# Three edits to a fused attention, soft MoE and ELU FFN kernel: how w1 is cut into loads, the order of the head's loads, and the order of the slots' softmax

## The chip, the cores and the metric

The kernel runs on one core of one Trainium2 chip. The metric is device time in microseconds (us), median of three runs. A profiled execution of the same kernel supplies the trace that is read below.

## The reference: what is computed

Three stages follow one another. Every array is float32.

```python
# 1: recurrent linear attention, B=4, H=8, S=768, D=48
for t in range(S):
    cur = np.einsum('bhd,bhe->bhde', u[None] * kt, vt)
    y[:, :, t] = np.einsum('bhd,bhde->bhe', rt, state + cur)
    state = w[None, :, :, None] * state + np.einsum('bhd,bhe->bhde', kt, vt)
# 2: soft MoE over x = y as [3072, 384]; 8 experts of 4 slots, w1[e] is 384x1024, w2[e] 1024x384
logits = x @ phi                       # [3072, 32]
d = softmax(logits, axis=0); slot_input = d.T @ x
h = np.maximum(slot_input[e] @ w1[e], 0.0); slot_out[e] = h @ w2[e]
x = softmax(logits, axis=1) @ slot_out
# 3: x @ w_in (384x2048), ELU, @ w_out (2048x384)
```

## The kernel before

**Attention.** The sequence is cut into 6 chunks of 128 tokens and each chunk into 4 units, one per batch entry, so there are 24 units. For each unit GpSimd (POOL) scales k into `k_nat` and makes the products r·u·k, TensorE (PE) turns k and r (`turn_k`, `turn_r`), makes scores, state terms and values, VectorE (DVE) evacuates with the decay tables, ScalarE (ACT) writes diagonals and y. Engines are synchronised by semaphores written by hand, and each engine runs its instructions in the order of the code.

**Loads.** Nearly all loads are issued by SyncE (SP) on one queue, called q1 in the profile, in program order. r, k and v come in rows of 48 numbers (192 bytes): each `load` call issues three transfers, one of 192 KB over 128 partitions and two of 96 KB over 64. `load_chunk` issues, for each half chunk, v, then k and r of the next chunk, then one piece of w1 (`load_w1`). w1 of one expert is 128 rows of 12 KB, one row to each partition: before the change it is cut across the row, into an 8 KB piece (two thirds, 1 MB) and a 4 KB piece (one third, 512 KB), both over all 128 partitions. The eight large pieces are loaded during attention, two small ones in the head, and the six others in the last chunk. Behind these, on the same queue, come w2 (`load_w2`, eight loads of 1.5 MB), w_in (two loads) and w_out (four). The profile shows w1 as `w_sb`, w2 as `w`.

**Head.** Before the first unit, w is loaded into `wcol`, raised to powers by repeated squaring in `wpow`, and `tables_T` holds w^t and w^-t. `wpow[:, 6]` is w^64 and `wpow[:, 7]` is w^128.

**Slots' softmax.** The softmax over the 3072 tokens runs in a turned layout. Chunks 0 to 4 are exponentiated early, with the maximum so far; the last chunk gets a new maximum (`neg_top[:, 1]`), its own exponentials `exp_T`, and a rescale of the earlier sum. PE turns the maxima (line 799) and `exp_T` (line 806), sums weighted tokens with `slot_in(c)`, and after `den_cols`, `fold_w` and `slot_parts` comes `slot_T`, which the experts' first matmul (`expert_in`, line 826) reads. It also waits for all of w1.

**FFN.** `expert_out` waits for w2 expert by expert; `G_first` and `G_others` multiply the 32 slots by w_in (line 903 needs w_in's second piece), ACT rounds w_out (line 1387), `move_G` moves parts of G_T from one group of 32 partitions to another, and a long stretch of matmuls (lines 976 to 978) ends the kernel.

Of the kernel before, what the change touches and what calls it, by code (L numbers as in the profile page):

```python
# [36 lines left out]
def attention_moe_ffn_kernel(nc, r, k, v, w, u, phi, w1, w2, w_in, w_out, out):  # L37
# [22 lines left out]
    with ExitStack() as ctx:  # L60
# [68 lines left out]
        logits_T = place("logits_T", [P, CHUNKS, P], F32)  # L129
# [86 lines left out]
        ps_warm = banks[5][:, 0:P]  # L216

# [174 lines left out]
        def _(sp):  # L392
# [44 lines left out]
            load_w1(range(2), slice(2, KD))  # L437
# [151 lines left out]
        def _(pe):  # L589
# [399 lines left out]
        def _(dve):  # L989
# [10 lines left out]
            for n in range(6):  # L1000
# [3 lines left out]
                dve.tensor_tensor(wpow[:, n + 1, :, :], wpow[:, n, :, :], wpow[:, n, :, :], ALU.mult).then_inc(powers, 1)  # L1004
# [46 lines left out]
            def logits_T_to_sbuf(c):  # L1051
# [5 lines left out]
                dve.tensor_copy(logits_T[:, c, :], logits_now[:, :]).then_inc(lT_kept, 1)  # L1057
# [88 lines left out]
            def row_weights(units):  # L1146
# [14 lines left out]
            logits_to_sbuf(CHUNKS - 1)  # L1161
# [5 lines left out]
            dve.wait_ge(exp_turned, 2)  # L1167
            dve.tensor_copy(col_w[:, EARLY_CHUNKS * B:UNITS, :].rearrange("p b s -> p (b s)"), banks[1][:, P:2 * P]
                            ).then_inc(col_w_ready, 1)
            dve.wait_ge(act_step, A_FOLD)  # L1170
            dve.tensor_tensor(fold_w[:, 1, :], fold_w[:, 1, :], fold[:, :], ALU.mult).then_inc(dve_step, 1)
            row_inverses(EARLY)
# [4 lines left out]
                              banks[3][:, DM:DM + 1].broadcast_to([P, P]), ALU.add).then_inc(dve_step, 1)  # L1177
            dve.tensor_tensor(slot_parts[:, :, :], *(x[:, 0:DM].rearrange("p (q c) -> p c q", c=KD) for x in (slot_early, banks[3])),
# [13 lines left out]

# [273 lines left out]
```

## Time and profile before

| | |
|---|---|
| median of 3 runs | 394.32 us (394.05 to 395.26) |
| profiled execution, its own time | 392.18 us |
| its span in the trace | 390.4 us |
| PE busy | 374.2 us (96%) |
| DVE, ACT, POOL busy | 69%, 56%, 26% |
| HBM read | 45.86 MB |
| granted TensorE clock | 1.00 |

The profiled execution took 1.78 us beyond its span, and the median of the three runs is 2.14 us above the profiled execution. A wait is read from the timeline rows: what stands in brackets is how long the engine idled before the group of instructions, and what released it. The DMA view gives, for a stretch, packets, megabytes, and the time that packets took as a share of 16 engines times the stretch.

### The profile page before, as it was taken

Reading aid. Unit: us, or ns where it says so; the run is one execution under the profiler, and the core shown is the slowest. Engines: PE = TensorE matmul, PEld = TensorE weight load, DVE = VectorE, ACT = ScalarE, POOL = GpSimd, SP = SyncE. Lnnn points to the kernel's source line nnn. Section 1 sums busy time; section 2 is a strip of 40 time slices with the busy share of each in tenths; the row PEclk is TensorE's granted clock in tenths of the full one; section 3 lists DMA queues with packets and bytes.
Section 4 is the critical chain, followed back from the end, with each engine's and each line's share of the span. In section 5 each row is a group of like instructions: output and inputs, shape, how many; then the busy total and the mean of one; then the engine's idle time right before and its main releaser. Section 6 shows DMA issues by size and latency. Waiting matters only on the chain.

```text
span 390.4 us, 11439 instructions
## 1 busy us (share of the span) xinstructions
PE 374.2 (96%) x4373; PEld 333.0 (85%) x4373; DVE 267.6 (69%) x512; ACT 219.6 (56%) x498; POOL 103.3 (26%) x136
## 2 busy tenths in 40 slices
PE   6898999999889999999999999999999999999996
PEld 3787898989775454589999999999999999999996
DVE  4787788778767620699867767667777667776671
ACT  2896778777772131588564446444644464455441
POOL 7797777777640000355200000000000000000000
PEclk9999999999999999999999999999999999999999
DMA  7989899999999999920020002000200020002002
GB/s 152 254 151 186 199 234 233 227 255 254 235 303 426 430 432 403 373 64 2 0 83 1 2 0 81 0 0 0 81 0 0 0 81 0 0 0 82 2 2 81
DMA packets 87280, 51.80 MB, mean 133 GB/s; under 512 B 77776, under 2 KB 83024, under 8 KB 85200
## 3 DMA queue, kind: packets, MB, share of 16 engines
q1 hardware_dynamic: 82368, 50.21, 43.1%
q10 hardware_dynamic: 4880, 1.16, 1.4%
q8 instruction: 19, 0.31, 0.3%
q14 instruction: 13, 0.11, 0.1%
HBM read 45.86 MB, written 4.72 MB: 130 GB/s over the span
## 4 chain that ended last, share of the span: by engine, by line
PE 79%; DMA 10%; SPq 3%; issue 3%; ACT 3%; DVE 1%; POOL 1%; DVEq 0%; POOLq 0%; ACTq 0%
PE psum L976 17%; PE psum L978 17%; PE psum L977 17%; PE psum L911 6%; DMA w_out_raw<-in_moe_w_out_dram 4%; PE psum L603 4%; DMA r_raw<-in_r_dram 3%; PE psum L643 3%; PE psum L826 3%; PE psum L686 3%; PE psum L667 2%; PE psum L656 2%; PE psum L696 2%; DMA v_sb<-in_v_dram 1%; PE psum L703 1%
## 5 line engine op out<-in xcount | busy, mean ns | idle before, releaser
L978 PE MATMUL psum<-w_out_hi,elu_lo 128*128 128x384 f32 x372 | 125.8, 338 | 0.0
L976 PE MATMUL psum<-w_out_hi,elu_hi 128*128 128x384 f32 x372 | 125.7, 338 | 0.0
L977 PE MATMUL psum<-w_out_lo,elu_hi 128*128 128x384 f32 x372 | 125.3, 337 | 0.0
L1405 ACT ACTIVATE exp_h<-psum 128x512 f32<-128x512 f32 x96 | 57.6, 600 | 97.3 <-PE psum L911 97.0
L1246 DVE SCALAR_TENSOR_TENSOR elu<-psum,neg_part 128x512 f32<-128x512 f32 x96 | 66.3, 690 | 57.1 <-ACT neg_part L1392 57.1
L977 PEld LDWEIGHTS psum<-w_out_lo,elu_hi 128*128 128x128 f32 x372 | 69.8, 188 | 3.9
L976 PEld LDWEIGHTS psum<-w_out_hi,elu_hi 128*128 128x128 f32 x372 | 70.4, 189 | 0.0
L978 PEld LDWEIGHTS psum<-w_out_hi,elu_lo 128*128 128x128 f32 x372 | 69.9, 188 | 0.0
L1238 DVE TENSOR_TENSOR elu_lo<-elu,elu_hi 128x512 fp32r<-128x512 f32 x96 | 66.3, 691 | 0.6
L1280 ACT ACTIVATE scores<-ident_wide,bonus 128x128 f32<-128x128 f32 x192 | 58.8, 390 | 5.0 <-DVE bonus L1028 4.9
L1392 ACT ACTIVATE neg_part<-exp_h 128x512 f32<-128x512 f32 x96 | 60.0, 626 | 1.7 <-DVE elu L1246 1.3
L1259 DVE CAST elu_hi<-elu 128x512 fp32r<-128x512 f32 x96 | 44.0, 458 | 0.6
L1041 DVE COPY_PREDICATED scores<-mask,psum 128x512 f32<-128x512 uint32 x48 | 33.3, 736 | 15.3 <-PE psum L643 12.9
L911 PE MATMUL psum<-c_T,G_T 128*128 (+1 forms) x96 | 37.6, 397 | 0.8 <-DMA G_T<-G_parts 0.6
L686 PE MATMUL psum<-scores,v_sb 64*64 64x128 f32 (+1 forms) x768 | 25.9, 245 | 1.8 <-issue 1.6
L527 POOL TENSOR_TENSOR k_nat<-k_raw,k_table 128x384 f32<-128x384 f32 x23 | 23.2, 1009 | 15.6 <-PE psum L667 7.9
L584 POOL TENSOR_TENSOR w_out_lo<-w_out_raw,w_out_hi 128x384 fp32r<-128x384 f32 x16 | 16.8, 1058 | 34.4 <-ACT w_out_hi L1387 34.4
L686 PEld LDWEIGHTS psum<-scores,v_sb 64*64 64x64 f32 x768 | 22.4, 133 | 2.8 <-issue 2.8
L538 POOL TENSOR_TENSOR k_raw<-k_raw,r_raw 128x384 f32<-128x384 f32 x22 | 22.1, 1006 | 6.0 <-DMA r_raw<-in_r_dram 4.7
L643 PE MATMUL psum<-r_pair,k_pair 48*64 48x128 f32 (+1 forms) x768 | 20.9, 245 | 1.8 <-DVE r_pair L1035 1.8
L535 POOL TENSOR_TENSOR k_raw<-k_raw,u_row 128x384 f32<-128x384 f32 x22 | 22.1, 1006 | 1.7
L911 PEld LDWEIGHTS psum<-c_T,G_T 128*128 128x128 f32 x96 | 18.1, 190 | 3.5 <-issue 1.7
(155 smaller groups left out, 403.6 us busy)
## 6 DMA issues: line engine op xcount, KB each, us to landing
w<-in_moe_w_dram SPq DMA_DIRECT2D x8, 1536.0 KB, 13.6
w_sb<-in_moe_w_dram SPq DMA_DIRECT2D x8, 1024.0 KB, 6.3
out_dram<-out_sb SPq DMA_DIRECT2D x24, 192.0 KB, 1.9
w_sb<-in_moe_w_dram SPq DMA_DIRECT2D x8, 512.0 KB, 6.2
w_out_raw<-in_moe_w_out_dram SPq DMA_DIRECT2D x4, 768.0 KB, 15.7
r_raw<-in_r_dram SPq DMA_DIRECT2D x12, 192.0 KB, 3.2
r_raw<-in_r_dram SPq DMA_DIRECT2D x24, 96.0 KB, 3.4
w_in_sb<-in_moe_w_in_dram SPq DMA_DIRECT2D x1, 2304.0 KB, 19.4
```

Source lines behind the costliest of these rows:

```text
L686: m = pe.matmul(ps_y[e * HP:e * HP + HP, two, q * P + cols.start:q * P + P], v_sb[rows, q, b, 2 * e + two, :], scores[rows, i, h, cols], s ...
L911: pe.matmul(banks[4 + f % RING][:, :], G_T[:, f * P:(f + 1) * P], c_T[:, bass.ds(i * BANK, BANK)], start=True, stop=True).then_inc(ffn_don ...
L976: pe.matmul(acc, hi, w_out_hi[:, f, :], start=(f == 0), stop=False)
L977: pe.matmul(acc, hi, w_out_lo[:, f, :], start=False, stop=False)
L978: m = pe.matmul(acc, lo, w_out_hi[:, f, :], start=False, stop=(f == KF2 - 1))
L1041: dve.copy_predicated(scores[:, i, two::2, :].rearrange("p (n a) t -> p n a t", n=2), mask[:, :, :].bitcast(U32).unsqueeze(2).broadcast_to ...
L1238: dve.tensor_tensor(elu_lo[:, f % RING, :], elu[:, f % 2, :], elu_hi[:, f % RING, :].bitcast(F32), ALU.subtract).then_inc(lo_done, 1)
L1246: dve.scalar_tensor_tensor(out=elu[:, f % 2, :], in0=banks[4 + f % RING][:, :], scalar=0.0, in1=neg_part[:, f % 2, :], op0=ALU.max, op1=AL ...
L1259: dve.tensor_copy(elu_hi[:, f % RING, :], elu[:, f % 2, :]).then_inc(hi_done, 1)
L1280: m = act.activation(scores[:, i, h, :], ident if h < H // 2 else ident_swap, ACT.Copy, scale=bonus[:, i, h:h + 1])
L1392: act.activation(neg_part[:, f % 2, :], exp_h[:, f % 2, :], ACT.Relu, bias=1.0, scale=-1.0).then_inc(neg_ready, 1)
L1405: act.activation(exp_h[:, f % 2, :], banks[4 + f % RING][:, :], ACT.Exp).then_inc(exp_done, 1)
```

## The change

There are three edits.

- **w1's pieces.** `load_w1` takes rows (partitions) instead of thirds. The first piece of an expert is partitions 0 to 79 with the whole 12 KB row (960 KB), the second partitions 80 to 127 (576 KB). Where they are issued, and in what number, stays.
- **The head.** SP issues u_row and then r; ACT issues the two loads of w, its table load and k, then v ahead of phi. Before, SP issued w and then r, and ACT k, u, phi and v. w^64 is written to PSUM (`w64`) instead of `wpow[:, 6]`; a copy of it and one more wait come ahead of w^128.
- **The slots' softmax.** PE turns `exp_T` right behind the maxima and moves the last chunk's turned logits (`chunk_logits`) behind `slot_in(5)`; DVE evacuates the exponentials first and moves the last logits and `row_inverses(EARLY)` behind `slot_T`; `exp_T` reads `logits_now` and the copy into `logits_T` is not made for the last chunk; on ACT `slot_early` goes ahead of the exponential of `fold_w`.

```diff
-            def load_w1(experts, thirds):
+            def load_w1(experts, rows):
                 for e in experts:
-                    sp.dma_start(w1_sb[:, e * KD + thirds.start:e * KD + thirds.stop, :], w1_dram[e][:, thirds, :]
-                                 ).then_inc(w1_loaded, 16)
+                    sp.dma_start(w1_sb[rows, e * KD:(e + 1) * KD, :], w1_dram[e][rows, :, :]).then_inc(w1_loaded, 16)
...
-                        load_w1([2 * (c - 1) + g], slice(0, 2))
+                        load_w1([2 * (c - 1) + g], slice(0, 5 * P // 8))
                     if last and g == 0:
-                        load_w1(range(2, E), slice(2, KD))
-            sp.wait_ge(cleared, 1)
-            for half in range(2):
-                sp.dma_start(wcol[half * HP:half * HP + D, :], w_cols, allow_slow_non_contiguous=True
-                             ).then_inc(w_loaded, 16)
+                        load_w1(range(2, E), slice(5 * P // 8, P))
+            sp.dma_start(u_row[:, :, :].rearrange("p h d -> p (h d)"), u_flat.broadcast_to([P, DM])).then_inc(u_loaded, 16)
             load_r(0, 0)
...
-            load_w1(range(2), slice(2, KD))
+            load_w1(range(2), slice(5 * P // 8, P))
...
             pe.transpose(banks[0][0:1, 0:P], neg_top[:, 1:2], ident[:, :]).then_inc(pe_step, 1)
-            chunk_logits(CHUNKS - 1)
+            pe.wait_ge(exp_T_ready, 2)
+            pe.transpose(banks[1][:, P:2 * P], exp_T[:, :], ident[:, :]).then_inc(exp_turned, 1)
             slot_in(2)
+            slot_in(3).then_inc(x_used, 1)
...
             slot_in(5).then_inc(pe_step, 1)
+            chunk_logits(CHUNKS - 1)
             keep_clock_up(2)
-            pe.wait_ge(dve_step, D_DENCOLS)
+            pe.wait_ge(dve_step, D_FOLD)
...
-                dve.tensor_tensor(wpow[:, n + 1, :, :], wpow[:, n, :, :], wpow[:, n, :, :], ALU.mult).then_inc(powers, 1)
+                dve.tensor_tensor(wpow[:, n + 1, :, :] if n < 5 else w64, wpow[:, n, :, :], wpow[:, n, :, :], ALU.mult).then_inc(powers, 1)
...
-            dve.tensor_tensor(wpow[:, 7, 0, :], wpow[:, 6, 0, :], wpow[:, 6, 0, :], ALU.mult).then_inc(powers, 1)
+            dve.tensor_copy(wpow[:, 6, 0, :], w64[:, 0, :]).then_inc(powers, 1)
+            dve.wait_ge(powers, 16)
+            dve.tensor_tensor(wpow[:, 7, 0, :], wpow[:, 6, 0, :], w64[:, 0, :], ALU.mult).then_inc(powers, 1)
...
+            act.wait_ge(cleared, 1)
+            for half in range(2):
+                act.dma_start(wcol[half * HP:half * HP + D, :], w_cols, allow_slow_non_contiguous=True
+                              ).then_inc(w_loaded, 16)
+            act.wait_ge(cleared, 2)
+            act.activation(exp_warm[:, :], v_sb[:, 0, 0, 0, D:D + 1], ACT.Exp)
             load(act, k_raw, k_dram, 0, 0, k_loaded)
-            act.wait_ge(const_set, 5)
-            act.activation(exp_warm[:, :], ident[:, 0:1], ACT.Exp)
-            act.dma_start(u_row[:, :, :].rearrange("p h d -> p (h d)"), u_flat.broadcast_to([P, DM])).then_inc(u_loaded, 16)
...
+            load(act, v_sb, v_dram, 0, 0, v_loaded)
+            act.wait_ge(powers, 15)
+            act.copy(tables_T[:, 1, 2:PAIRS, 0:HP], tables_T[:, 1, 2:PAIRS, HP:P]).then_inc(table_swapped, 1)
```

SP's instructions in the order of the program, first the head, before the change (`w_sb` is w1, the last numbers are partitions x elements):

```order
L430 DMA wcol<-in_w_dram 48x8x1 x2
L375 DMA r_raw<-in_r_dram 128x8x48
L376 DMA r_raw<-in_r_dram 64x8x48
L377 DMA r_raw<-in_r_dram 64x8x48
L375 DMA k_raw<-in_k_dram 128x8x48
```

The same place on SP in the changed kernel:

```order
L429 DMA u_row<-in_u_dram 128x384
L377 DMA r_raw<-in_r_dram 128x8x48
L378 DMA r_raw<-in_r_dram 64x8x48
L379 DMA r_raw<-in_r_dram 64x8x48
L377 DMA k_raw<-in_k_dram 128x8x48
```

w has left SP's queue for ACT's, and u stands in its place; r is issued second as before.

SP in the last chunk and behind it, before:

```order
L377 DMA v_sb<-in_v_dram 64x8x48
L405 DMA w_sb<-in_moe_w_dram 128x1024 x6
L441 DMA w_0_84<-in_moe_w_dram 128x3072
L441 DMA w_1_85<-in_moe_w_dram 128x3072
L441 DMA w_2_86<-in_moe_w_dram 128x3072
```

And in the changed kernel:

```order
L379 DMA v_sb<-in_v_dram 64x8x48
L407 DMA w_sb<-in_moe_w_dram 48x3072 x6
L439 DMA w_0_84<-in_moe_w_dram 128x3072
L439 DMA w_1_85<-in_moe_w_dram 128x3072
L439 DMA w_2_86<-in_moe_w_dram 128x3072
```

The six pieces stand in the same place, ahead of w2. Their shape went from 128 partitions of 1024 numbers to 48 partitions of 3072.

PE in the slots' softmax, from the turned maxima to the experts, before:

```order
L799 MATMUL psum<-ident_wide,neg_top 1x128
L709 MATMUL psum<-ident_wide,logits_now 128x128
L725 MATMUL psum<-x_sb,col_w 32x386 x4
L803 MATMUL psum<-top_row,ones 128x32
L806 MATMUL psum<-ident_wide,exp_T 128x128
L725 MATMUL psum<-x_sb,col_w 32x386 x12
L593 MATMUL psum<-ones 128x128 x2
L812 MATMUL psum<-fold_w,den_cols 128x32
```

And in the changed kernel:

```order
L797 MATMUL psum<-ident_wide,neg_top 1x128
L799 MATMUL psum<-ident_wide,exp_T 128x128
L723 MATMUL psum<-x_sb,col_w 32x386 x8
L803 MATMUL psum<-top_row,ones 128x32
L723 MATMUL psum<-x_sb,col_w 32x386 x8
L707 MATMUL psum<-ident_wide,logits_now 128x128
L591 MATMUL psum<-ones 128x128 x2
L810 MATMUL psum<-fold_w,den_cols 128x32
```

The exponentials' turn moved ahead of all of `slot_in(2)` to `slot_in(5)`, and the logits' turn behind them; the number of matmuls is the same.

## Rows read from the trace of the kernel before

**Rows 1.** The page: granted clock and GB/s in 40 slices of 9.76 us

```profile
PEclk9999999999999999999999999999999999999999
...
GB/s 152 254 151 186 199 234 233 227 255 254 235 303 426 430 432 403 373 64 2 0 83 1 2 0 81 0 0 0 81 0 0 0 81 0 0 0 82 2 2 81
```

**Rows 2.** The chain that ended last: start us, us, what

```profile
77.74 5.56 DMA v_sb<-in_v_dram
...
93.25 4.04 DMA r_raw<-in_r_dram
...
102.86 4.50 DMA r_raw<-in_r_dram
...
144.50 16.14 DMA w_out_raw<-in_moe_w_out_dram
```

**Rows 3.** Timeline of SP's queue: start us, us, line, output<-input

```profile
66.77 0.62 SPq L405 DMA_DIRECT2D w_sb<-in_moe_w_dram  x1
...
103.54 0.66 SPq L405 DMA_DIRECT2D w_sb<-in_moe_w_dram  x1
...
107.77 5.94 SPq L405 DMA_DIRECT2D w_sb<-in_moe_w_dram  x6
```

**Rows 4.** Timeline of POOL in attention, with the idle time before it

```profile
76.40 1.01 POOL L527 TENSOR_TENSOR k_nat<-k_raw,k_table 128x384 f32<-128x384 f32 x1 [1.89 <-DMA k_raw<-in_k_dram]
```

**Rows 5.** The DMA view of 119 to 150 us: totals, share of 16 engines

```profile
DMA packets 1386, 13.21 MB, mean 426 GB/s; under 512 B 144, under 2 KB 144, under 8 KB 359
...
q1 hardware_dynamic: 1382, 13.15, 100.4%
```

**Rows 6.** The DMA view of 111.4 to 118.6 us, the last w1 pieces

```profile
DMA packets 740, 2.68 MB, mean 372 GB/s; under 512 B 91, under 2 KB 91, under 8 KB 738
```

**Rows 7.** The DMA view of 169.95 to 170.45 us, one G_T move, 40 slices

```profile
GB/s 0 0 0 164 492 328 164 0 164 164 328 0 328 328 164 0 328 492 655 164 164 0 0 164 164 0 164 0 164 1 2 164 0 0 0 1 0 0 0 0
...
q1 hardware_dynamic: 48, 0.07, 55.5%
```

**Rows 8.** The DMA view of 388 to 390.4 us, the last stores

```profile
q1 hardware_dynamic: 398, 0.54, 63.3%
```

**Rows 9.** Timeline where the FFN begins: start us, us, engine, line, operation

```profile
158.84 1.92 PE L903 MATMUL psum<-w_in_sb,slot_out_T 128*32 128x512 f32 x12 [0.66 <-DMA w_in_sb<-in_moe_w_in_dram]
...
160.67 0.93 ACT L1387 CAST w_out_hi<-w_out_raw 128x384 fp32r<-128x384 f32 x2 [2.62 <-DMA w_out_raw<-in_moe_w_out_dram]
```

**Rows 10.** Timeline of the head

```profile
0.95 1.03 SPq L430 DMA_DIRECT2D wcol<-in_w_dram  x2
...
2.02 0.47 SPq L375 DMA_DIRECT2D r_raw<-in_r_dram  x1
...
6.12 0.39 SPq L375 DMA_DIRECT2D k_raw<-in_k_dram  x1
...
7.53 0.15 DVE L1022 TENSOR_TENSOR wpow<-wpow 128x4 f32<-128x4 f32 x1
...
7.95 0.63 PE L603 MATMUL psum<-ident_wide,r_raw 128*128 128x128 f32 x4 [1.73 <-DMA r_raw<-in_r_dram]
...
17.75 0.51 POOL L566 TENSOR_TENSOR state<-state_sum,wpow 128x192 f32<-128x192 f32 x1
```

**Rows 11.** Timeline of the slots' softmax and after it

```profile
122.06 0.86 PE L725 MATMUL psum<-x_sb,col_w 128*32 128x386 f32 x8
...
123.18 0.33 PE L806 MATMUL psum<-ident_wide,exp_T 128*128 128x128 f32 x1
...
125.70 0.29 DVE L1176 TENSOR_TENSOR den_cols<-slot_early,psum 128x128 f32<-128x128 f32 x1 [0.42 <-PE psum L725]
...
127.97 3.59 PE L826 MATMUL psum<-w_sb,slot_T 128*32 128x512 f32 x29
...
131.99 1.75 DVE L1202 TENSOR_TENSOR row_parts<-row_w,row_hi 128x1536 fp32r<-128x1536 f32 x1
...
139.24 1.45 PEld L861 LDWEIGHTS psum<-ident_r,row_parts 128*128 128x128 f32 x16
```

More of the change, by code:

```diff
@@ L127, in attention_moe_ffn_kernel @@
         W1_END = cursor[0]
-        logits_T = place("logits_T", [P, CHUNKS, P], F32)
+        logits_T = place("logits_T", [P, CHUNKS - 1, P], F32)
         exp_T = place("exp_T", [P, P], F32)
@@ L216, in attention_moe_ffn_kernel @@
         ps_warm = banks[5][:, 0:P]
+        w64 = banks[1][:, 0:2 * PAIRS].rearrange("p (n a) -> p n a", n=2)
         h_banks = ((banks[3], banks[4]), (banks[0], banks[7]))
@@ L341, in attention_moe_ffn_kernel @@
         LOADED = 3 * 16
-        DECAY_SET = 16
+        DECAY_SET = 17
         PE_TOP_T, PE_TOP_ROWS, PE_SLOT_IN, PE_DEN, PE_SLOT_T = range(1, 6)
-        (D_TOP_ROW, D_FOLD_SHIFT, D_FOLD, D_DENCOLS, D_SLOT_PARTS, D_DENEPS, D_DENINV, D_SLOT_T,
+        (D_TOP_ROW, D_FOLD_SHIFT, D_DENCOLS, D_FOLD, D_SLOT_PARTS, D_DENEPS, D_DENINV, D_SLOT_T,
          D_ROWW, D_ROWW_LATE, D_ROWHI, D_PARTHI, D_PARTLO) = range(1, 14)
-        A_RESCALE, A_FOLD, A_EARLY_SLOTS, A_IDENT_R = range(1, 5)
+        A_RESCALE, A_EARLY_SLOTS, A_FOLD, A_IDENT_R = range(1, 5)
         def move_G(eng, n, j):
@@ L804, in _ @@
                       ).then_inc(pe_step, 1)
-            pe.wait_ge(exp_T_ready, 2)
-            pe.transpose(banks[1][:, P:2 * P], exp_T[:, :], ident[:, :]).then_inc(exp_turned, 1)
-            slot_in(3).then_inc(x_used, 1)
             slot_in(4).then_inc(early_slots_done, 1)
             slot_in(5).then_inc(pe_step, 1)
+            chunk_logits(CHUNKS - 1)
             keep_clock_up(2)
-            pe.wait_ge(dve_step, D_DENCOLS)
+            pe.wait_ge(dve_step, D_FOLD)
             pe.matmul(banks[0][:, 2 * P:2 * P + SLOTS], den_cols[:, :], fold_w[:, 1, :], start=True, stop=True
@@ L1014, in _ @@
                 dve.tensor_tensor(tables_T[:, n, pairs, 0:HP], tables_T[:, n, pairs, HP:P],
-                                  wpow[:, 6, 1 - n, pairs].unsqueeze(2).broadcast_to([P, pairs.stop, HP]), ALU.mult
+                                  w64[:, 1 - n, pairs].unsqueeze(2).broadcast_to([P, pairs.stop, HP]), ALU.mult
                                   ).then_inc(tables_done, 1)
@@ L1056, in logits_T_to_sbuf @@
                 dve.tensor_reduce(chunk_top[:, c:c + 1], logits_now[:, :], AX.X, ALU.max).then_inc(chunk_top_ready, 1)
-                dve.tensor_copy(logits_T[:, c, :], logits_now[:, :]).then_inc(lT_kept, 1)
+                if c < EARLY_CHUNKS:
+                    dve.tensor_copy(logits_T[:, c, :], logits_now[:, :]).then_inc(lT_kept, 1)
             def early_top():
@@ L1160, in _ @@
                               ).then_inc(dve_step, 1)
-            logits_to_sbuf(CHUNKS - 1)
+            dve.wait_ge(exp_turned, 2)
+            dve.tensor_copy(col_w[:, EARLY_CHUNKS * B:UNITS, :].rearrange("p b s -> p (b s)"), banks[1][:, P:2 * P]
+                            ).then_inc(col_w_ready, 1)
             dve.wait_ge(pe_step, PE_TOP_ROWS)
@@ L1166, in _ @@
                               ).then_inc(dve_step, 1)
[L1167 to L1172, printed above, removed]
             dve.wait_ge(pe_step, PE_SLOT_IN)
@@ L1177, in _ @@
                               banks[3][:, DM:DM + 1].broadcast_to([P, P]), ALU.add).then_inc(dve_step, 1)
+            dve.wait_ge(act_step, A_FOLD)
+            dve.tensor_tensor(fold_w[:, 1, :], fold_w[:, 1, :], fold[:, :], ALU.mult).then_inc(dve_step, 1)
             dve.tensor_tensor(slot_parts[:, :, :], *(x[:, 0:DM].rearrange("p (q c) -> p c q", c=KD) for x in (slot_early, banks[3])),
@@ L1191, in _ @@
                                   ).broadcast_to([P, KD, E, SPE]), ALU.mult).then_inc(dve_step, 1)
+            logits_to_sbuf(CHUNKS - 1)
+            row_inverses(EARLY)
             row_weights(EARLY)
@@ L1302, in _ @@
                                   ).then_inc(phi_loaded, 16)
-            act.wait_ge(powers, 15)
-            act.copy(tables_T[:, 1, 2:PAIRS, 0:HP], tables_T[:, 1, 2:PAIRS, HP:P]).then_inc(table_swapped, 1)
-            load(act, v_sb, v_dram, 0, 0, v_loaded)
             act.wait_ge(table_turned, 1)
@@ L1345, in _ @@
             act.wait_ge(top_ready, 2)
-            act.wait_ge(lT_kept, CHUNKS)
-            act.activation(exp_T[:, :], logits_T[:, CHUNKS - 1, :], ACT.Exp, bias=neg_top[:, 1:2]).then_inc(exp_T_ready, 1)
+            act.wait_ge(lT_ready, CHUNKS)
+            act.activation(exp_T[:, :], logits_now[:, :], ACT.Exp, bias=neg_top[:, 1:2]).then_inc(exp_T_ready, 1)
             act.activation(rescale[:, :], neg_top[:, 0:1], ACT.Exp, bias=neg_top[:, 1:2], scale=-1.0).then_inc(act_step, 1)
-            act.wait_ge(dve_step, D_FOLD_SHIFT)
-            act.activation(fold_w[:, 1, :], fold_w[:, 0, :], ACT.Exp).then_inc(act_step, 1)
             act.wait_ge(early_slots_done, 1)
@@ L1353, in _ @@
             act.activation(slot_early[:, :], banks[2][:, 0:DM + 2], ACT.Copy, scale=rescale[:, :]).then_inc(act_step, 1)
+            act.wait_ge(dve_step, D_FOLD_SHIFT)
+            act.activation(fold_w[:, 1, :], fold_w[:, 0, :], ACT.Exp).then_inc(act_step, 1)
             act.wait_ge(rows_shifted, 2)
```

2 lines of the change are left out of this document (1 added, 1 removed).

## The prediction, made before the changed kernel was timed

> **What bounds the kernel now.** I began with the page's slices [rows 1]: the granted clock is full (2.4 GHz) all through, and from the 12th slice to the 17th the DMA moves 303 to 432 GB/s. The chain that ended last [rows 2] tells where that matters. It runs through a load of w_out from 144.50 us, 16.14 us long, which ends when the FFN can begin, and during attention through v and r. So I split the kernel in three.
>
> Until about 107 us it is attention. Its second half runs to the beat of SP's queue: w1's pieces are issued at 66.77 and, four pieces later, at 103.54 [rows 3], so 9.2 us for half a chunk, and POOL waits for k at each (1.89 us in the row shown, and four waits like it from 67 to 104 us) [rows 4]. In this stretch, time that a w1 piece takes on the queue delays the k, r and v behind it.
>
> From 107.77 us, when the last six pieces of w1 are issued [rows 3], the queue is full. From 111.4 to 118.6 us it moves 372 GB/s in 4 KB rows [rows 6], then 426 GB/s in the 12 KB rows of w2 [rows 5]. w_in's second piece and w_out's first end the stage: PE waits 0.66 us for the one and ACT 2.62 us for the other, until 160.67 us [rows 9]. Every microsecond that the queue loses between 111 and 160 us is a microsecond of the kernel. The softmax and the experts lie beside it; after 160.67 us PE is busy to the end, and nothing of the change is there.
>
> **w1's pieces, last stage.** The six second pieces go from 6 x 0.524 = 3.15 MB over 128 partitions to 6 x 0.590 = 3.54 MB over 48. Before, at 372 GB/s [rows 6], they cost 8.5 us. What does a transfer cost that lands in a part of the partitions? The nearest rows are the moves of G_T, 64 KB from 32 partitions to 32. One fills slices 4 to 32 of 40, 29 x 0.0125 = 0.36 us, so 181 GB/s while it runs [rows 7], though all 16 engines share it. Its packets took 55.5% x 16 x 0.5 us = 4.44 us of engine time for 65.5 KB, or 14.8 GB/s per engine. The last stores, in packets of 1.5 KB over 128 partitions, took 63.3% x 16 x 2.4 = 24.3 us for 0.54 MB, or 22.2 GB/s per engine [rows 8]; w2 took 100.4% x 16 x 31 = 498 us for 13.15 MB, or 26.4 GB/s per engine [rows 5]. The shorter packets of the stores are faster than those of G_T, so the length does not explain it: few partitions do. The bounds for 3.54 MB are then 8.3 us (426 GB/s, no loss), 15.0 us (G_T's engine rate, 16 x 14.8 = 236), 19.6 us (181) and 22.1 us (160, which is 426 in proportion to 48 of 128 partitions). The last two are the nearest in kind, since the first ignores the row and the second leaves out that the engines wait unevenly. I take 21 us: **+12.5**.
>
> The Trainium skill speaks against this edit: SBUF — State Buffer, section Door 1: The DMA port swizzle, says that the partitions hang on 16 ports of 27.2 GB/s, eight to each, and that a range of partitions gets only the ports it reaches. By its map, four ports hold eight of the partitions 80 to 127 each, so a piece would need 8 x 12 KB / 27.2 GB/s = 3.6 us and six 21.7 us, which is an estimate from that page; the sum would be 0.7 us higher. The G_T moves agree with it, at 181 GB/s against its 218 for 32 partitions; no run before shows an HBM load of this shape.
>
> Who waits: w1 would be complete near 111 + 21 + 2 = 134 us instead of 111 + 8.5 = 119.5, so `expert_in`, which began at 127.97 [rows 11], begins some 6 us late. w2 is queued behind and later by 12.5, so PE waits for each expert, and w_in and w_out arrive 12.5 later.
>
> **w1's pieces in attention.** The eight first pieces go from 1.049 MB (2.5 us at 426) to 0.983 MB over 80 partitions: 2.3 us without loss, 3.7 us at 80/128 of the rate (266 GB/s), so between -0.2 and +1.2 us each. At 181 GB/s, G_T's own, it would be 5.4 us, +2.9; I take +1.2, since 80 partitions are far more than 32. From 66.77 to 103.54 us there are these four beats that the queue sets [rows 3, 4], so +4.9 there; the earlier pieces have slack or half of it. In the head the two second pieces cost 2 x 2.2 us more of queue time at 14 to 20 us, where PE has its data well ahead; I put 0 there, up to +2. With a little taken back by later slack: **+5** (from -1 to +9).
>
> **The head.** r's issue moves from 2.02 us to about 1.3, since SP no longer waits for w's two issues of 1.03 us, but k's on ACT moves back by about the same, behind them. PE's first turn needs r (landed at 7.9 us) and its second k, which released SP at 6.12 [rows 10]. The bytes ahead of both are the same, so both land near 7.4: **-0.3**, between -0.8 and +0.8. w^64 in PSUM, its copy and one wait touch a chain that ends at 7.53 + 0.15 us, while POOL needs w^128 at 17.75 [rows 10]: 0. Without that cover it would be the copy, about 0.15 us, like the product in that row.
>
> **The softmax.** PE turned `exp_T` at 123.18, between `slot_in(2)`, which began at 122.06, and the other three [rows 11]; now it does so about 1 us sooner, but the four `slot_in` that follow take 0.86 us for the first and as much or less for each of the others, and there was hardly a gap between them. `den_cols` at 125.70 comes at best 0.5 us sooner. `row_parts`, 1.5 us later because `row_inverses` moved behind `slot_T`, would be ready at 131.99 + 1.75 + 1.5 = 135.2 against PE's use at 139.24 [rows 11]. All this lies beside the queue: **0**. If that cover were gone it would be worth -0.5.
>
> **Sum.** 392.18 (the profiled execution) + 12.5 + 5 - 0.3 = 409.4; the median lies 2.1 above the profiled one, so 411.5 us.
>
> **The rivals.**
> - *No loss by partitions* (0.16). G_T's packets also come out of 32 partitions of SBUF and are 2 KB; a load from HBM in 12 KB rows might not care. Then the last stage gains 8.5 - 8.3 = 0.2, attention loses 0.066 MB a beat, -0.15 to -0.3 each over four beats, and the head gives -0.3: 394.3 - 1.5 = 392.8. Faster decides from where 3.54 MB move at more than 3.54 / 9.8 = 361 GB/s, as the other gains are 1.3. For it speaks that 4 KB rows moved at 372 and 12 KB rows at 426 [rows 5, 6]; against it rows 7 beside rows 8. Of this, faster has 0.11 and same 0.05.
> - *Half of it* (0.12). The queue's engines run on without waiting for one another, so those with light rows take w2 early, and the price is G_T's engine rate: last stage 15.0 - 8.5 = +6.5, attention +2, head -0.3: 402.5. Against it: w_in and w_out need the slowest engine.
> - *The clock falls as well* (0.10). PE, busy all through now at full clock [rows 1], would wait for w2 expert by expert. If it were granted 1.2 GHz at the start of the FFN, line 903's 1.92 us and what follows until the first G_T moves would double, +3 to +5: 415.5. No row here is at that level.
>
> The forecast itself has 0.62, its own range 404 to 417.
>
> **How the numbers follow.** About 0.3% is what a measurement of this kernel can tell from no change. The range 398 to 419 holds the forecast, the half case and most of the clock case, 0.62 + 0.12 + 0.08, and leaves out the case without loss. Faster 0.11, same 0.05, slower 0.84.
>
> **What would show it.** In the profile after, w1's last pieces land 3.5 us apart and the GB/s fall to 150 to 200 from 111 to 132 us; PE waits for w1 before line 824 and then for w2; the beat of SP's pieces goes from 9.2 to 10.4 us; w_out lands near 178 us. If instead the GB/s stay at 400 behind the last v, the first rival is right and the prediction is wrong. If the softmax matters, PE's wait for w_in would have to be gone.

## The result and the profile after

The changed kernel takes 426.15 us (median of four runs, 424.39 to 428.64) against 394.79 us of the kernel before beside it: the ratio is 1.086, with an interval of 1.079 to 1.092. It is 31 us slower, 15 us more than forecast and outside the range.

The page of the changed kernel, granted clock and GB/s in 40 slices, here of 10.65 us, beside [rows 1]:

```profile
PEclk9988989989998799999999999999999999999999
...
GB/s 133 182 143 152 197 176 182 204 204 206 205 186 176 148 255 430 424 410 357 42 0 0 77 0 2 71 2 0 0 74 0 0 61 13 0 0 75 1 2 74
```

The queue is at 206 GB/s or less up to the 14th slice, where before it moved 227 to 303 from the 6th to the 12th. The clock, full before in every slice, drops under 90% in six of the first 14. From the 16th slice the rates are those of before.

The chain that ended last, beside [rows 2]:

```profile
24.74 5.58 issue
...
50.70 4.07 issue
...
71.17 6.39 DMA v_sb<-in_v_dram
...
91.99 6.62 DMA v_sb<-in_v_dram
...
133.08 24.25 DMA w_sb<-in_moe_w_dram
157.37 10.51 PE psum L824 x96
...
173.89 22.05 DMA w_out_raw<-in_moe_w_out_dram
```

New are two long stretches "issue", in which PE waited for nothing that the chain names (before, the longest was 1.38 us), and 24.25 us for w1. The wait for w_out went from 16.14 to 22.05 us.

SP's queue, beside [rows 3], with the first, the fourth and the eighth of the large pieces:

```profile
19.67 6.67 SPq L377 DMA_DIRECT2D r_raw<-in_r_dram  x1
...
44.07 1.13 SPq L407 DMA_DIRECT2D w_sb<-in_moe_w_dram  x1
...
79.65 0.34 SPq L407 DMA_DIRECT2D w_sb<-in_moe_w_dram  x1
...
122.90 0.62 SPq L407 DMA_DIRECT2D w_sb<-in_moe_w_dram  x1
...
125.81 7.69 SPq L407 DMA_DIRECT2D w_sb<-in_moe_w_dram  x6
```

[rows 3] has the fourth, at 66.77, and the eighth, at 103.54; the first stood here before:

```profile
35.92 0.62 SPq L405 DMA_DIRECT2D w_sb<-in_moe_w_dram  x1
```

The last six pieces are issued at 125.81 us instead of 107.77: **18.0 us** are lost by then. 8.2 of them are lost by the first large piece. From the first to the fourth it is three half chunks of 11.86 us (before 10.28), 4.7 us more; from the fourth to the eighth four of 10.81 us (before 9.19), 6.5 us more. Behind the eighth 1.3 us come back.

The end of the stage, beside [rows 9]:

```profile
157.37 10.51 PE L824 MATMUL psum<-w_sb,slot_T 128*32 128x512 f32 x96 [0.55 <-DMA w_sb<-in_moe_w_dram]
...
195.96 0.93 ACT L1392 CAST w_out_hi<-w_out_raw 128x384 fp32r<-128x384 f32 x2 [2.74 <-DMA w_out_raw<-in_moe_w_out_dram]
```

From the six pieces to this row it is 70.15 us instead of 52.90: **17.25 us** more. From it to the end it is 229.9 us, before 229.7. So the loss is 18.0 + 17.25 = 35.3 us, the difference of the spans (425.9 - 390.4 = 35.5; this profiled run took 427.61 us, the one of before 392.18, so they lie 4 us further apart than the medians).

The DMA view of 134 to 156 us, when the last w1 pieces move, and the same stretch by windows (PE, PEld, DVE, ACT, POOL busy, granted clock, DMA share, GB/s):

```profile
DMA packets 365, 3.46 MB, mean 157 GB/s; under 512 B 84, under 2 KB 84, under 8 KB 84
...
q1 hardware_dynamic: 363, 3.43, 99.0%
...
134.00:156.00 22.00, 15.60 (x199) 9.39 (x192) 7.07 (x17) 3.95 (x9) 0.82 (x1) 0.77 1.00 157
```

The DMA engines are busy 99% of the time, as with w2 before [rows 5], but move 157 GB/s instead of 426: their packets take longer. PE is busy for 15.60 of these 22 us. It idles only 0.55 us for w1; its long gap is another one, a stop of 6.11 us in the middle of a group:

```profile
146.73 1.08 PE L701 MATMUL psum<-y_T,phi_sb 128*32 128x128 f32 x15 [6.11 <-issue]
```

The granted clock averages 0.77 in the window (0.50 in the 2.3 us behind this stop), and 1.00 between 156 and 190 us. PE's 96 products for the experts take 10.51 us in both timelines, so here this fall of the clock cost them nothing.

The middle of the head and the first chunk, timeline rows with the idle time before them:

```profile
23.97 0.78 PE L641 MATMUL psum<-r_pair,k_pair 48*64 48x128 f32 x22
...
30.32 0.58 PE L641 MATMUL psum<-r_pair,k_pair 48*64 48x64 f32 x10 [5.58 <-issue]
...
30.13 1.00 POOL L525 TENSOR_TENSOR k_nat<-k_raw,k_table 128x384 f32<-128x384 f32 x1 [7.12 <-DMA k_raw<-in_k_dram]
```

PE stops after 22 of 32 matmuls of one group, without a wait that the trace names, and goes on 5.58 us later. The kernel before has one such stop above 1 us, 1.38 us at 32.65 us. POOL meanwhile waits for k.

### The profile page after: what moved, and what is told of

It is laid out like the page before. It is cut to its first block, busy times and chain, and to the rows that moved or that the text cites. A ratio compares the mean times of both kernels' runs of the same rounds, so it can differ in the third digit from the quotient of the medians.

```text
span 425.9 us, 11439 instructions
## 1 busy us (share of the span) xinstructions
PE 384.7 (90%) x4373; PEld 339.3 (80%) x4373; DVE 266.2 (62%) x512; ACT 219.7 (52%) x498; POOL 103.4 (24%) x136
## 3 DMA queue, kind: packets, MB, share of 16 engines
HBM read 45.86 MB, written 4.72 MB: 119 GB/s over the span
## 4 chain that ended last, share of the span: by engine, by line
PE 67%; DMA 17%; SPq 7%; issue 4%; POOL 2%; DVE 1%; ACT 1%; ACTq 0%; POOLq 0%; DVEq 0%
PE psum L974 15%; PE psum L976 15%; PE psum L975 15%; DMA w_sb<-in_moe_w_dram 6%; DMA w_out_raw<-in_moe_w_out_dram 5%; PE psum L909 5%; DMA v_sb<-in_v_dram 3%; PE psum L601 3%; SPq L377 3%; PE psum L824 2%; PE psum L641 2%; SPq L407 2%; PE psum L684 2%; SPq L378 2%; PE psum L665 2%
## 5 line engine op out<-in xcount | busy, mean ns | idle before, releaser
L1041 DVE COPY_PREDICATED scores<-mask,psum 128x512 f32<-128x512 uint32 x48 | 32.9, 734 | 27.2 <-PE psum L641 26.5
L684 PE MATMUL psum<-scores,v_sb 64*64 64x128 f32 (+1 forms) x768 | 27.3, 255 | 2.4 <-DMA v_sb<-in_v_dram 1.7
L641 PE MATMUL psum<-r_pair,k_pair 48*64 48x128 f32 (+1 forms) x768 | 21.9, 248 | 6.6 <-issue 5.6
L684 PEld LDWEIGHTS psum<-scores,v_sb 64*64 64x64 f32 x768 | 24.0, 141 | 3.7 <-issue 3.7
L641 PEld LDWEIGHTS psum<-r_pair,k_pair 48*64 48x64 f32 x768 | 19.4, 136 | 7.4 <-issue 7.2
L1276 ACT COPY k_pair<-psum 128x512 f32<-128x512 f32 x23 | 13.4, 584 | 19.9 <-PE psum L601 19.8
## 6 DMA issues: line engine op xcount, KB each, us to landing
w<-in_moe_w_dram SPq DMA_DIRECT2D x8, 1536.0 KB, 22.1
```

Of the source, the lines that this page charges most:

```text
L641: m = pe.matmul(ps_A[two][e0:e0 + HP, a, cols], k_pair[rows, i, a, e0:e0 + HP], r_pair[rows, i, a, cols], start=True, stop=True, skip_grou ...
L684: m = pe.matmul(ps_y[e * HP:e * HP + HP, two, q * P + cols.start:q * P + P], v_sb[rows, q, b, 2 * e + two, :], scores[rows, i, h, cols], s ...
```

## The experiments

Each was run beside the kernel before. All that differ in w1 alone are named "w1 edit alone" and keep the head and the softmax of before. The diffs of experiments 3, 4 and 7 are against the w1 edit alone, that of 5 against the cut at 64, that of 8 against the new head alone, the others against the kernel before. A profile is one execution, and single profiles scatter by some 2 us at a given row (experiment 2, softmax), so smaller differences in such rows aren't read as effects.

**1. Loads alone.** All computation is left out, and the output is zeros. Eight series of w1 loads and two of v, each awaited before the next; of the third:

```diff
...
+            for e in range(E):
+                sp.dma_start(w1_sb[80:128, e * KD:(e + 1) * KD, :], w1_dram[e][80:128, :, :]).then_inc(landed[2], 16)
+            sp.wait_ge(landed[2], 16 * E)
...
```

> This kernel leaves out all of the computation: it only issues series of eight loads of w1 into SBUF, waits for each series, then v's rows, then stores zeros. Each series is eight loads on SP's queue. Theory P (the partitions set the rate: a transfer gets a share of the way into SBUF by the partitions it lands in): 128 partitions run at about 425 GB/s with 12 KB rows and 370 to 410 with 4 KB rows; partitions 80 to 127 at 160 to 180 GB/s (8 x 0.59 MB in 26 to 29 us); partitions 0 to 79 at 210 to 270; 0 to 63 at 210 to 220; 0 to 31 at 180 to 220, so hardly less than 0 to 63; every other partition, also 64 of them but spread over all, clearly over 0 to 63, 300 to 425; 4 KB rows into partitions 80 to 127 also near 165. Rival R (the 12 KB row is what costs): whole experts over 128 partitions are as slow as the partial ones, and 4 KB rows into 48 partitions are fast. Rival N (the number of partitions counts, wherever they lie): every other partition is as slow as 0 to 63, and 0 to 31 takes half the rate of 0 to 63. For v's rows of 192 bytes P expects no difference between 128 partitions and two halves of 64.

SP's queue: each series of eight loads ends where the next begins.

```profile
2.14 3.97 SPq L250 DMA_DIRECT2D w_sb<-in_moe_w_dram  x8
14.90 3.98 SPq L254 DMA_DIRECT2D w_sb<-in_moe_w_dram  x8
47.13 3.65 SPq L258 DMA_DIRECT2D w_sb<-in_moe_w_dram  x8
81.34 3.81 SPq L262 DMA_DIRECT2D w_sb<-in_moe_w_dram  x8
118.08 5.09 SPq L266 DMA_DIRECT2D w_sb<-in_moe_w_dram  x8
151.00 4.99 SPq L270 DMA_DIRECT2D w_sb<-in_moe_w_dram  x8
168.65 3.57 SPq L274 DMA_DIRECT2D w_sb<-in_moe_w_dram  x8
185.73 3.57 SPq L278 DMA_DIRECT2D w_sb<-in_moe_w_dram  x8
197.63 13.43 SPq L282 DMA_DIRECT2D v_sb<-in_v_dram  x6
213.28 18.78 SPq L288 DMA_DIRECT2D v_sb<-in_v_dram  x12
234.40 12.17 SPq L294 DMA_DIRECT2D out_dram<-out_sb  x24
```

| series, partitions and row | MB | us | us a load | GB/s |
|---|---|---|---|---|
| L250: 0 to 127, 4 KB | 4.19 | 12.76 | 1.60 | 329 |
| L254: 0 to 127, 12 KB | 12.58 | 32.23 | 4.03 | 390 |
| L258: 80 to 127, 12 KB | 4.72 | 34.21 | 4.28 | 138 |
| L262: 0 to 79, 12 KB | 7.86 | 36.74 | 4.59 | 214 |
| L266: 0 to 63, 12 KB | 6.29 | 32.92 | 4.12 | 191 |
| L270: every other, 12 KB | 6.29 | 17.65 | 2.21 | 356 |
| L274: 0 to 31, 12 KB | 3.15 | 17.08 | 2.14 | 184 |
| L278: 80 to 127, 4 KB | 1.57 | 11.90 | 1.49 | 132 |

The times hold the start and the landing of a series, 1.4 to 2.3 us in which no w1 packet moves. The DMA views without them give 407 GB/s for 0 to 127, 147 for 80 to 127, 223 for 0 to 79, 206 for 0 to 63, 394 for every other and 207 for 0 to 31.

Sixty-four neighbouring partitions and sixty-four alternate ones have the same size of row, bytes and count, and differ by a factor of 1.9. So it is the place of the partitions, with the rows of w1 in HBM that belong to them: no run moves the one without the other, but the whole experts, read from neighbouring rows as well, aren't slow. A load of 48, 64 or 80 neighbouring partitions takes as long as one of all 128: **either piece of an expert costs as much as the whole expert**, 4.59 + 4.28 against 4.03 us. The 4 KB row is as slow by the byte as the 12 KB one (132 and 138 GB/s). So rivals R and N are out, and theory P has the order right, but several of its figures were too high (80 to 127: 138 instead of 160 to 180), and with v it failed: six loads of its 192-byte rows over 128 partitions, each awaited, take 15.65 us, and the same bytes as two halves of 64 take 21.12 us. Whether the place or the second load of each pair costs this isn't separated.

The Trainium skill, SBUF — State Buffer, section Door 1: The DMA port swizzle, has this pattern: each of the four sets 0 to 63, 0 to 79, 80 to 127 and 0 to 127 has some port with eight of its partitions, for which an estimate from that page's port rate is 8 x 12 KB / 27.2 GB/s = 3.6 us, and every other partition or 0 to 31 puts four on a port, 1.8 us by the same estimate. The runs agree in the order, and lie 12 to 27% above (4.03 to 4.59, and 2.14 to 2.21); without the start and the landing of the series it is 5 to 21% (3.83 to 4.38, and 1.90 to 1.99). It is the fullest port that fits, not the section's own rule of 27.2 GB/s for each port that a range reaches: that would be an estimate of 218 GB/s for 80 to 127 (eight ports) and 326 for 0 to 79 (twelve), against 147 and 223 in the DMA views.

**2. One edit at a time.** The kernel before with one of the three edits, each as in the diff of the change; of the first one:

```diff
-                        load_w1([2 * (c - 1) + g], slice(0, 2))
+                        load_w1([2 * (c - 1) + g], slice(0, 5 * P // 8))
```

> The kernel before with the edit to w1's pieces alone. If w1's pieces carry the whole loss, 424 us, within 2 of the changed kernel's 426.15, the granted clock again near 0.97, and PE idle for some 5 us in the third slice of 9.8 us. If the head and the softmax carry a part of it (rival H), 415 to 421 us.

> The kernel before with the new head alone (loads' order and w^64 in PSUM). In the changed kernel PE's first turn of r began at 9.27 us instead of 7.95, with w landed 1.6 us later. Theory: the new order itself does that, +1.3 us at the first turn, of which attention gives back some: 394.8 to 396.2 us. Rival: the late start is an accident of that one execution and the prediction's -0.3 holds: 394.0 to 394.5.

> The kernel before with the new order of the slots' softmax alone. The queue of w2, w_in and w_out ends the stage, so the forecast is no change, 394.3 plus or minus 0.5, with w_out landing at 160.7 as before although the experts begin up to 0.5 us sooner. Rival: the softmax lets w2's later loads be issued sooner and gives 0.5 us or more.

w1 alone: 424.26 us, ratio 1.084 (1.077 to 1.092). Head alone: 394.91 us, 1.010 (1.003 to 1.018). Softmax alone: 393.62 us, 1.002 (0.998 to 1.006), no change (its profiled run, 395.92, is the slowest of ten and has w_out at 164.38 us, not 160.7). The w1 edit carries the loss.

**3. Bytes moved, width kept.** The w1 edit alone, with the same 983 and 590 KB in each piece, but cut by columns over all 128 partitions.

```diff
-                    sp.dma_start(w1_sb[rows, e * KD:(e + 1) * KD, :], w1_dram[e][rows, :, :]).then_inc(w1_loaded, 16)
+                    sp.dma_start(w1_sb[:, :, :].rearrange("p (e c) f -> p e (c f)", e=E)[:, e, cols], w1_dram[e].rearrange("p c f -> p (c f)")[:, cols]).then_inc(w1_loaded, 16)
```

> The w1 edit alone with the same bytes in each piece (983 KB first, 590 KB last), but cut by columns over all 128 partitions: rows of 7.5 and 4.5 KB. Theory A, the loss is the partitions': no loss, the last six cost 0.39 MB more than before at about 400 GB/s, +1 us, attention -0.5: 394 +- 2 us. Theory B, that moving bytes from the first to the last pieces, or pieces that aren't whole rows of a third, costs it: over 400 us.

392.86 us, ratio 1.002 (0.998 to 1.005). Last pieces issued at 106.27 us (-1.5), from there to w_out 54.06 us (+1.2). Theory A: the split of the bytes costs nothing that this can tell.

**4. Half of the partitions, neighbouring or alternate.** The w1 edit alone, two kernels, of each the line of the first pieces (the last pieces take the other 64 partitions):

```diff
-                        load_w1([2 * (c - 1) + g], slice(0, 5 * P // 8))
+                        load_w1([2 * (c - 1) + g], slice(0, P // 2))
```

```diff
-                        load_w1([2 * (c - 1) + g], slice(0, 5 * P // 8))
+                        load_w1([2 * (c - 1) + g], slice(0, P, 2))
```

> The w1 edit alone, cut at partition 64 instead of 80: first pieces in partitions 0 to 63, last ones in 64 to 127, 786 KB each, the same count and the same 12 KB rows. In the loads alone 0 to 63 took 4.1 us each (191 GB/s) against 4.5 for 0 to 79 and 4.2 for 80 to 127. Theory A, the adjacent partitions share ways into SBUF: as slow as the cut at 80, beats of 10 to 11 us, the last six pieces about 24 us, 418 to 428 us in all. Theory B, it is the uneven cut, 5 to 3, that leaves some ways idle: the even cut gives back at least half of the loss, under 410 us.

> The w1 edit alone, but the first piece of an expert is its even partitions and the last its odd ones: 64 partitions, 786 KB, the same 12 KB rows and the same number of pieces as with the cut at 64. Theory A, place alone matters: 356 GB/s in the loads alone, so 2.2 us for a piece; the first pieces have 262 KB less than before (-0.6 us a beat over four beats, -2), the last six 1.57 MB more than before (4.72 MB at 356 = 13.3 us against 8.5, +4.8): 393 to 398 us, the granted clock back at 1.00 and the stalls of PE with the releaser issue under 1.5 us. Theory B, that few partitions or rows of 12 KB in a part of the tile are slow wherever they lie: over 415 us, as with the cut at 64.

Neighbouring: 418.42 us, ratio 1.069 (1.062 to 1.076). Alternate: 393.98 us, 1.005 (1.002 to 1.008). Clock and GB/s of the alternate cut:

```profile
PEclk9998999999999999999999999999999999999999
...
GB/s 151 254 162 172 195 222 217 233 243 204 229 363 425 426 431 407 383 82 2 0 82 2 2 0 80 0 0 0 80 0 0 0 80 0 0 0 82 2 2 80
```

Against 155 to 208 GB/s of the neighbouring cut in slices 3 to 14, this is nearly the kernel before. With rows, bytes and counts of the same size the place is worth 24 us. PE has one stop above 1 us, 1.60 us, slightly over the 1.5 expected. The 1.57 MB more in the last stage fit what remains of 0.5%: the issue comes at 105.78 us (-2.0), w_out 2.95 us later than before from there.

In the cut at 64 the clock had a price: the 96 products of the experts begin at 147.29 us, run at a granted clock of 0.50 until 152 us, and take 13.46 us instead of 10.51.

**5. Does a neighbour in the queue fill the idle ways?** The cut at 64, with the next piece in the opposite half.

```diff
-                        load_w1([2 * (c - 1) + g], slice(0, P // 2))
+                        load_w1([2 * (c - 1) + g], slice(g * HP, g * HP + HP))
...
-                        load_w1(range(2, E), slice(P // 2, P))
+                        for e in range(2, E):
+                            load_w1([e], slice((1 - e % 2) * HP, (1 - e % 2) * HP + HP))
```

> The cut at partition 64 as in the run of that cut (418.4 us), but neighbours in the queue lie in opposite halves: of an even expert the first piece is 0 to 63 and the last 64 to 127, of an odd one the other way round. Theory A, the engines stay on the same piece, so it is narrow whatever its neighbour: 416 to 421 us. Theory B, the engines run a piece or more apart, so that opposite halves fill all the ways: the last six go from 24 us towards the 13.3 of every other partition, the head's two pieces too, and the kernel takes 398 to 410 us.

418.79 us, ratio 1.065 (1.059 to 1.071), the same as without. From the last six pieces to w_out it is 68.36 us, against 68.79. Theory A: a neighbour in the other half gives nothing back.

**6. The two stages apart.** The kernel before, with wide pieces issued as two halves of 64 partitions, in attention only, or in the last stage only.

```diff
+                    for half in halves:
+                        sp.dma_start(w1_sb[half, e * KD + thirds.start:e * KD + thirds.stop, :],
+                                     w1_dram[e][half, thirds, :]).then_inc(w1_loaded, 16)
...
```

> The kernel before with one change: each of the eight first pieces of w1 (two thirds, 1.05 MB) is issued as two halves, partitions 0 to 63 and then 64 to 127; the head's and the last stage's pieces stay wide. 1.05 MB at the 191 GB/s of partitions 0 to 63 are 5.5 us against 2.5. Theory A, that the narrow pieces in attention and those in the last stage each cost for themselves: the last six pieces are issued 9 to 18 us later than 107.8, the time from there to w_out stays at 53 us, 402 to 411 us in all. Theory B, that the two halves overlap in the queue, or that attention has room: under 398 us.

> The kernel before with one change: the last six pieces of w1 (one third each, 3.15 MB) are issued as all six lower halves (partitions 0 to 63) and then all six upper halves. At 191 GB/s 16.5 us instead of 8.5. Theory A, that every microsecond which the queue loses here is one of the kernel: attention as before (last pieces issued at 107.8 us), the time from there to w_out 61 us instead of 53, 400 to 403 us in all, and the granted clock falls in the last stage without a price in the experts' products. Theory B, that part of it is hidden by w2's slack or the engines run ahead: under 398 us.

Attention only: 409.0 us, ratio 1.042 (1.035 to 1.048); last pieces issued at 122.38 us (+14.6), from there 54.2 us. Last stage only: 400.67 us, 1.018 (1.012 to 1.024); issued at 108.39 us (+0.6), from there 60.0 us (+7.1, by the loads alone 3.15 MB / 191 - 8.5 = +8.0). Each stage pays for itself; both kernels also have more loads (16 instead of 8, and 12 instead of 6), while experiment 4 keeps the number. In the second, a window of the stage (columns as above):

```profile
122.00:130.00 8.00, 5.75 (x49) 2.53 (x52) 2.63 (x11) 1.33 (x4) 0.00 (x0) 0.79 1.03 264
130.00:140.00 10.00, 9.83 (x96) 4.75 (x92) 8.38 (x19) 1.68 (x4) 0.00 (x0) 1.00 1.00 421
```

PE stands in another stop until 124.25 us (2.82 us); the clock is 0.50 from there to 126, 0.64 to 128 and 1.00 afterwards. So it falls behind the stop and is back before the experts' products, which take 10.51 us.

**7. The stops of PE in the middle of a group.** First, the w1 edit alone with the first two experts in thirds over 128 partitions again.

```diff
-                        load_w1([2 * (c - 1) + g], slice(0, 5 * P // 8))
+                        if c == 1:
+                            load_w1_thirds([2 * (c - 1) + g], slice(0, 2))
+                        else:
+                            load_w1([2 * (c - 1) + g], slice(0, 5 * P // 8))
...
-            load_w1(range(2), slice(5 * P // 8, P))
+            load_w1_thirds(range(2), slice(2, KD))
```

> The w1 edit alone (424.3 us), but the first two experts in thirds over 128 partitions as before, so that the pieces issued in the head and in the first chunk are wide; experts 2 to 7 stay rows of 12 KB in partitions 0 to 79 and 80 to 127. Theory A, that PE's stalls in the middle of a matmul group (3.38, 2.70 and 7.48 us with the releaser issue) are instruction fetches standing in the queue's engines behind narrow pieces: the first of them, at about 23 us, goes (under 1.5 us, as the 1.38 us before), the first chunk's products come near 30 us instead of 35, the later ones stay, and the kernel takes 415 to 420 us. Theory B, that the stalls have another cause: the stall at 23 us stays above 2.5 us and the kernel takes over 421 us.

415.97 us, ratio 1.060 (1.054 to 1.067). The stop at 23 us is gone, the first product with phi comes at 30.86 us instead of 35.34, and the last pieces are issued at 116.53 instead of 122.10. But two beats of attention have wide pieces here too. So the pieces were moved and nothing else:

```diff
+                    if first and g == 1:
+                        load_w1(range(2), slice(5 * P // 8, P))
...
             load_v(0, 1)
-            load_w1(range(2), slice(5 * P // 8, P))
```

> The w1 edit alone (424.3 us), but the head's two narrow pieces are issued behind the k and r of the second half of the first chunk, about 15 us later. Theory A, that the stall of PE in the middle of a matmul group is a transfer of instructions that stands behind narrow packets: the stall at 23 us (3.38 us) falls under 1 us, PE's first product with phi comes at 30 to 31.5 us instead of 35.3, and a stall of 2 us or more appears where the pieces now are, at 30 to 45 us; the kernel takes 418 to 424 us, since part of the cost has moved with them. Theory B, that the stall belongs to that place of the program: it stays at 23 us with 2.5 us or more.

424.27 us, ratio 1.082 (1.076 to 1.089). The timeline of PE:

```profile
29.93 1.08 PE L703 MATMUL psum<-y_T,phi_sb 128*32 128x128 f32 x32
...
32.43 0.27 PE L686 MATMUL psum<-scores,v_sb 64*64 64x128 f32 x1
39.84 0.92 PE L686 MATMUL psum<-scores,v_sb 64*64 64x128 f32 x15 [7.13 <-issue]
```

The first chunk is back at its time of before (29.93 against 29.88 us), the stop at 23 us has gone, and one of 7.13 us stands where the pieces now are, in the group in which the kernel before stops for 1.38 us. The total is as without the move, 0.3 us above what was expected: the cost has moved with the pieces. The DMA view of 36.5 to 39.8 us of this run:

```profile
q1 hardware_dynamic: 3213, 0.60, 108.8%
q8 instruction: 1, 0.02, 2.2%
```

From 32.7 to 36.5 us the same view lists no transfer of instructions, only q1. So one lands in the second part of the stop, and PE goes on after it. Theory A: the stop follows the narrow pieces.

The other traces bear this out. In the 14 with computation PE has 29 stops of 1 us or more that have the releaser "issue", and **each of the 29 ends 1.2 to 1.8 us behind the end of a 16 KB packet of queue q8, the one of instructions**. In the changed kernel these packets end at 28.88, 53.30 and 144.99 us, and PE goes on at 30.32, 54.77 and 146.73. The stops are 2.7 to 7.5 us long in the w1 edit alone, where before, with columns, with alternate partitions, and with the head or the softmax alone none is above 2.0 us. With halves in attention only they reach no more than 1.9 us, and with halves in the last stage only 2.8, so narrow pieces alone don't set their length. So PE waited for instructions, as far as the times can tell. That their packets come late because the engines hold narrow ones follows from the edits, not from a row: no view shows a packet waiting.

**8. The head.** The new head alone, u's load behind r's.

```diff
-            sp.dma_start(u_row[:, :, :].rearrange("p h d -> p (h d)"), u_flat.broadcast_to([P, DM])).then_inc(u_loaded, 16)
             load_r(0, 0)
+            sp.dma_start(u_row[:, :, :].rearrange("p h d -> p (h d)"), u_flat.broadcast_to([P, DM])).then_inc(u_loaded, 16)
```

> The new head alone (394.9 us, PE's first product at 8.94 us), but u's load of 196 KB on SP stands behind the first r instead of ahead of it. Theory A, u ahead of r delays r and k: PE's first product comes before 8.3 us, and the time is that of before within 0.3 per cent. Theory B, it is w, whose two loads of single elements now stand ahead of k on ACT: the first product stays at 8.7 to 9.0 us and the ratio stays near 1.01.

395.15 us, ratio 1.006 (1.002 to 1.009). Its timeline:

```profile
6.12 0.63 PE L602 MATMUL psum<-ident_wide,r_raw 128*128 128x128 f32 x4
...
8.52 0.66 PE L625 MATMUL psum<-ident_wide,k_raw 64*48 64x64 f32 x32 [1.77 <-DMA k_raw<-in_k_dram]
```

r is turned at 6.12 us, earlier than before (7.95), so u ahead of it was one cause (theory A). But k, behind w on ACT, comes at 8.5 us, and SP, which waits for it, issues the next k at 8.49 instead of 6.12: neither theory alone. The interval of the ratio overlaps that of the new head (1.010), so how much of the 1% u carries stays open. The 0.55% also lies over the 0.3% that theory A allowed.

| kernel | first chunk at | second at | last six issued | from there to w_out |
|---|---|---|---|---|
| before | 29.88 | 49.98 | 107.77 | 52.90 |
| after | 38.62 | 62.44 | 125.81 | 70.15 |
| w1 edit alone | 35.34 | 56.39 | 122.10 | 70.09 |
| cut by columns | 29.87 | 50.26 | 106.27 | 54.06 |
| first two experts in thirds | 30.86 | 51.23 | 116.53 | 69.78 |
| pieces later | 29.93 | 56.05 | 120.67 | 69.09 |
| cut at 64 | 36.46 | 56.56 | 117.67 | 68.79 |
| cut at 64, opposite halves | 36.48 | 56.90 | 118.84 | 68.36 |
| every other partition | 34.02 | 52.26 | 105.78 | 55.85 |
| halves in attention only | 30.14 | 52.66 | 122.38 | 54.23 |
| halves in the last stage only | 31.09 | 50.64 | 108.39 | 59.98 |
| head alone | 31.93 | 52.03 | 108.83 | 54.15 |
| head alone, u behind r | 31.22 | 52.10 | 108.83 | 52.51 |
| softmax alone | 29.75 | 50.44 | 109.34 | 55.04 |

The first two columns are the starts in us of PE's products with phi of chunks 0 and 1, from the timeline; the last two are from rows like those of SP and ACT above.

## Why the prediction was wrong

The direction was right, and so was the mechanism, that loads into part of the partitions are slow. The place wasn't: attention, which had 5 of the 17.2 us, lost 18.0 of the 35.3, and the last stage, which had 12.5, lost 17.25.

- **Attention, +5: the steps that failed are "I put 0 there, up to +2"**, for the head's two narrow pieces, and **"the earlier pieces have slack or half of it"**. 8.2 us are lost by the first large piece. The argument was that PE has its data well ahead; but SP's issue of r stood still for 6.67 us (before 2.90), POOL waited 7.12 us for k, and PE stopped for 5.58. In the w1 edit alone the head's pieces make the first product with phi 5.4 us late: it comes at 35.34 us, and at 29.93 when they alone are moved (experiment 7; before 29.88). The head edit alone costs 2.1 us there. In the changed kernel it is 8.7 us (38.62), so 1.2 us appear only with both, and no run shows why. Then the three half chunks that were given slack cost 4.7 us, with a stop of PE of 4.07 us in them. The four that were priced at +1.2 each, +4.9, took +1.6 each, +6.5.
- **Each first piece at 3.7 us.** Alone it takes 4.59 us, 2.1 more than the 2.5 of the old piece, and the half chunk took up 1.6 of that. I took the rate in proportion to 80 of 128 partitions; the runs show no such proportion, since 64 neighbouring partitions take as long as all 128.
- **The last stage, +12.5: the mis-sized term is the 21 us for six pieces.** The stage measured +17.25. The pieces took 4.28 us each alone, 25.7 us for six; 25.7 - 8.5 = 17.2. Even the largest bound, 22.1 us, was too small, since it has 426 GB/s in proportion to 48 partitions. The nearest row, G_T, gave 181 GB/s for 32 partitions; 32 neighbouring ones gave 184 in the loads alone. What it did not tell is that 48 can be slower in GB/s than 32.
- **The head, -0.3.** It measured +1% alone, and in the changed kernel:

```profile
6.06 0.19 ACT L1301 COPY wpow<-wcol 64x4 f32<-64x4 f32 x1 [2.65 <-DMA wcol<-in_w_dram]
...
9.27 0.63 PE L601 MATMUL psum<-ident_wide,r_raw 128*128 128x128 f32 x4 [2.06 <-DMA r_raw<-in_r_dram]
...
9.54 0.38 SPq L377 DMA_DIRECT2D k_raw<-in_k_dram  x1
```

  Beside [rows 10], r is turned 1.3 us later and the next k issued 3.4 us later. "The bytes ahead of both are the same" was false: u, 196 KB, had been issued at 2.99 us, behind k and r's first two loads, and went ahead of r. Experiment 8 shows r's part; that k is late because w stands ahead of it is read from the order of issues.
- **The softmax, 0.** Right.
- **The rivals.** No loss by partitions, and half of it, are out. "The clock falls as well" was right that it falls, but not in its place: in the changed kernel the experts and the FFN take the same time. In attention, the groups behind a stop are slower: the granted clock is 0.50 from 30.3 to 35.1 us, and in the chain a group that takes 1.02 us elsewhere takes 1.90 and 1.47 us. With the groups beside them that is about 3 us behind the two stops.
- **What would show it.** Last pieces at 150 to 200 GB/s: 157. The beat 10.4 us: 10.8. Pieces 3.5 us apart: 4.3 alone. PE's wait for w1: there, but only 0.55 us. w_out near 178 us: 195.96. What was not on the list are PE's stops.

## What to carry to other kernels

Cut a load across the row, or take alternate partitions, but not a range of neighbouring partitions: a range of 48 to 80 took as long as all 128. If a queue is slow in a stretch, what stands behind on its engines is late too, and by the reading of experiment 7 that includes the instructions, which no load in the program asks for; so "PE has its data ahead" doesn't make that stretch free. And when one row of a trace gives the rate of a shape, ask what sets it before it is scaled by the number of partitions.

## What the runs showed of the hardware that was not expected

- 48 neighbouring partitions (80 to 127) load at 138 GB/s, slower than 32 (0 to 31, 184 GB/s), and 80 take longer than 128 (4.59 against 4.03 us a load).
- Pieces in opposite halves of the partitions, one behind the other on a queue, gain nothing (68.36 against 68.79 us from the last six to w_out).
- Narrow pieces in the queue stop PE in the middle of a group for 2.7 to 7.5 us (w1 edit alone), where the kernel before stops for 1.38 at most. All 29 stops of 1 us or more, in 14 traces, end 1.2 to 1.8 us behind a 16 KB packet of the instruction queue.
